# Expert attention: the low-part product of the two widest query tiles made in the two row halves of the array

## The reference

```
def _moe2_ref(x, w_gate, wq, wk, wv, wo):
    ...
    for e in range(E):                       # E = 4, for both batches
        q = x @ wq[e]
        k = x @ wk[e]
        v = x @ wv[e]
        scores = scale * (q @ k.transpose(0, 2, 1))
        causal = np.triu(np.ones((S, S), dtype=bool), 1)
        scores = np.where(causal, -1000000000.0, scores)
        scores = scores - scores.max(-1, keepdims=True)
        a = np.exp(scores)
        a /= a.sum(-1, keepdims=True) + 1e-09
        ye = a @ v @ wo[e]
        ...
```

## Time and profile before

| | before |
|---|---|
| median of three runs | 709.78 us (708.51 to 711.83) |
| the profiled execution: its time / its span | 710.88 us / 709.0 us |
| TensorE busy (matmuls) | 677.2 us (96%), 3808 instructions |
| VectorE busy | 356.4 us (50%), 828 |
| ScalarE busy | 393.9 us (56%), 800 |
| GpSimd busy | 273.9 us (39%), 244 |
| granted TensorE clock, mean | 0.998 of full speed (2.4 GHz), no slice lower than 9 tenths |

### The profile page before, as it was taken

The page is one execution under the profiler, slowest core; times in us unless marked ns, Lnnn a source line. Parts: engine busy times, 40 slices in busy tenths (PEclk is TensorE's granted clock), DMA queues, the critical chain, the costliest instruction groups (busy, mean ns, idle before and its releaser), DMA issues. The chain is left out here.

```text
span 709.0 us, 11959 instructions
## 1 busy us (share of the span) xinstructions
PE 677.2 (96%) x3808; PEld 538.7 (76%) x3808; DVE 356.4 (50%) x828; ACT 393.9 (56%) x800; POOL 273.9 (39%) x244
## 2 busy tenths in 40 slices
PE   6899999999999989999999999999999979999987
PEld 5677676677676737888888888888888968788866
DVE  5787778788788736111121111211112667786482
ACT  4777777777777746323343333433333656676574
POOL 6355454555444021444544444444443012232020
PEclk9999999999999999999999999999999999999999
DMA  4222111232120892000000000000000000000102
GB/s 150 61 92 86 60 63 61 64 105 65 60 63 16 239 306 60 0 0 0 0 1 0 0 0 0 0 0 0 0 0 1 30 1 1 0 1 31 60 2 89
DMA packets 26923, 31.34 MB, mean 44 GB/s; under 512 B 9664, under 2 KB 20880, under 8 KB 26896
## 3 DMA queue, kind: packets, MB, share of 16 engines
q1 hardware_dynamic: 26896, 31.01, 14.0%
HBM read 26.75 MB, written 3.15 MB: 42 GB/s over the span
## 5 line engine op out<-in xcount | busy, mean ns | idle before, releaser
L911 DVE SCALAR_TENSOR_TENSOR hid_l<-psT,hid_h 128x512 fp32r<-128x512 f32 x48 | 33.2, 692 | 212.1 <-ACT hid_h L887 212.1
L935 POOL TENSOR_TENSOR w_l<-w_raw,w_h 128x512 fp32r<-128x512 f32 x48 | 62.0, 1291 | 134.5 <-ACT w_h L878 134.5
L436 ACT ACTIVATE probs<-psS,scale_bias 128x768 f32<-128x768 f32 x96 | 95.2, 992 | 33.3 <-DVE scale_bias L522 32.8
L512 DVE TENSOR_REDUCE negmax<-psS 128x1 f32<-128x768 f32 x96 | 91.6, 954 | 30.2 <-PE psS L343 27.6
L356 PE MATMUL psT<-ident,probs 128*128 128x128 f32 x576 | 83.5, 276 | 3.7 <-ACT pt L445 1.8
L878 ACT ACTIVATE w_h<-w_raw 128x512 fp32r (+1 forms) x48 | 30.3, 631 | 95.2 <-PE psS L844 95.2
L356 PEld LDWEIGHTS psT<-ident,probs 128*128 128x128 f32 x576 | 66.6, 140 | 20.4 <-issue 9.6
L342 PE MATMUL psS<-k_hh,q_lh 128*128 128x384 f32 x192 | 73.9, 385 | 5.0 <-ACT probs L436 2.8
L833 PE MATMUL psT<-x_h,w_h 128*128 x192 | 74.8, 390 | 0.7 <-DVEq L903 0.7
L833 PE MATMUL psT<-x_l,w_h 128*128 x192 | 74.8, 389 | 0.0
L833 PE MATMUL psT<-x_h,w_l 128*128 x192 | 74.8, 389 | 0.0
(11 more groups left out here) (192 smaller groups left out, 1388.2 us busy)
## 6 DMA issues: line engine op xcount, KB each, us to landing
raw<-qk SPq DMA_DIRECT2D x15, 768.0 KB, 4.5
w_raw<-w SPq DMA_DIRECT2D x16, 256.0 KB, 6.7
w_raw<-w SPq DMA_DIRECT2D x4, 1024.0 KB, 8.6
raw_v<-v_n SPq DMA_DIRECT2D x16, 192.0 KB, 2.3
out<-y_out SPq DMA_DIRECT2D x11, 256.0 KB, 2.0
raw<-qk SPq DMA_DIRECT2D x2, 384.0 KB, 3.9
q_hb<-bits SPq DMA_DIRECT2D x30, 18.0 KB
k_lb<-bits SPq DMA_DIRECT2D x30, 18.0 KB
```

Of the source, the lines that this page charges most:

```text
L436: nc.scalar.activation(probs[j % 3][:].rearrange("p (c n) -> p c n", c=2), psS[:, score_slot(p, j), :, 0:HALF], ACT.Exp, bias=scale_bias[: ...
L512: nc.vector.tensor_reduce(negmax[:, p, j:j + 1], psS[:, score_slot(p, j), :, 0:HALF], AXIS.XY, ALU.max, negate=True).then_inc(rowmax_ready, 1)
L935: nc.gpsimd.tensor_tensor(w2_l[s][:].rearrange("p a b -> p (a b)"), w2_raw[:, f, :], w2_h[s][:].rearrange("p a b -> p (a b)").bitcast(F32) ...
```

## The change

For heads 1 to 7 and tiles 4 and 5, the products with `k_ll` no longer run over all 128 rows, twice in succession. The one for the first 512 keys uses rows 0 to 63 alone (high q times low k), and right behind it the one for the other 256 keys uses rows 64 to 127 alone, written to the second bank. The built instructions are placed in the array's upper and lower row half (64 x 128 each). Since rows 64 to 127 of `q_hl` hold the low part of q, a copy of the rounded q is made for these rows: `q_low`, 384 tokens (tiles 3 to 5), one more ScalarE instruction at the head of `round_qk` for c = 1. The product of the two low parts, which the 128-row form added for these tiles, is left out. Head 0, whose q comes from the stage before, and tiles 0 to 3 stay as they were.

```diff
@@ expert_attention
         summed = sb("esummed", [P, QT, D])
+        q_low = [sb(f"eq_low{p}", [P, HALF], F32R) for p in range(2)]
...
@@ scores
                         ps = psS[:, slot, c, 0:k.stop - k.start]
-                        nc.tensor.matmul(ps, q_hl[p][:, q], k_ll[p][:, k], start=True, stop=False)
+                        if j < 4 or h == 0:
+                            nc.tensor.matmul(ps, q_hl[p][:, q], k_ll[p][:, k], start=True, stop=False)
+                        elif c == 0:
+                            nc.tensor.matmul(ps, q_hl[p][0:D, q], k_ll[p][0:D, k], start=True, stop=False)
+                            other = slice(512, max(768, width))
+                            nc.tensor.matmul(psS[:, slot, 1, 0:other.stop - 512], q_low[p][D:P, q.start - HALF:q.stop - HALF],
+                                             k_ll[p][D:P, other], start=True, stop=False)
                         here = j // 4 == c
                         last = nc.tensor.matmul(ps, q_hl[p][:, q], k_hh[p][:, k], start=False, stop=not here)
...
@@ round_qk
                     act.wait_ge(qk_ready, 2 * (h - 1) + c + 1)
+                    if c == 1:
+                        nc.scalar.activation(q_low[h % 2][D:P, :], psS[0:D, c, 1, 0:HALF], ACT.Copy, scale=SCALE)
                     round_projection(nc, c, psS, q_hl[h % 2], k_hh[h % 2], False).then_inc(qk_rounded, 1)
```

## The result

| | before | after |
|---|---|---|
| median (lowest to highest) | 711.25 us (708.51 to 712.39), 13 runs | 714.06 us (712.91 to 718.25), 13 runs |
| the profiled execution: time / span | 710.88 / 709.0 us | 714.06 / 712.2 us |
| TensorE busy | 677.2 us, 3808 instructions | 680.3 us, 3808 |
| ScalarE busy | 393.9 us, 800 | 398.1 us, 807 |

The ratio is 1.0044, with the interval 1.0026 to 1.0062: slower by 3.1 us, or by 2.8 between the medians. The forecast was 711.3 us, in a range from 708.3 to 713.8; the measured median lies 0.3 us above that range.

The account below looks back on a forecast made before the run. VectorE was taken to bound heads 1 to 4 and 6, tile 4 and 5 score products heads 5 and 7. Terms 0.85 + 0.2 + 0.5 = +1.5 us gave 711.3 us from the median, range 708.3 to 713.8.

Parts of the forecast that it names:

- the starting point: Whole kernel: the +1.5 us sum was carried from the profiled execution's 710.88 us to the median of 709.78.
- the copy: ScalarE, heads 1 to 7: one added 0.49 us copy, mostly hidden by idle time; +0.5 us, 0.4 of it in head 0.
- the tiles: TensorE, tiles 4 and 5: +0.85 us at four exposed tiles in heads 5 and 7, +0.2 us in five VectorE-bound heads.
- without overlap: Rival: the row halves run one after the other in tiles 4 and 5, the gain absent; 712.8 us, chance 0.13.
- a full stop: Rival: TensorE drains at each change of shape in tiles 4 and 5, 0.58 us per tile; 717.0 us, chance 0.10.
- The slack of 0.42 us: ScalarE's idle time before tile 1's copy in head 3, said to hide all but 0.07 us of the added copy.
- The shape's round trip: TensorE, tiles 4 and 5: full array to halves and back, taken as 0.33 us from the hashed attention's column halves.
- the columns saved: TensorE, tiles 4 and 5: the 256-column product vanishes behind the 512-column one, saving 0.115 us per tile.
- The 0.2 for the five other heads: VectorE-bound heads: tile 4 fits 0.23 us of idle time, tile 5 overruns by 0.05 each; +0.2 us.
- the halves' start within 0.05 us: Sign in the profile after: the 256-column half product starts less than 0.05 us after the 512-column one.
- tile 5's 0.8 to 0.95 us in head 3: Sign: time from first low product to transposes; 0.75 if the shape change is free, over 1.2 at a stop.
- wrong if head 3 grows by over 0.3 us: Test refuting the forecast, alongside tiles 4 and 5 of head 5 getting shorter.

Follow-up runs that it names:

- e4: Kernel before plus only the added ScalarE copy, written to the rows it was read from (0 to 63); 711.1 against 710.62 us, ratio 1.0007.
- e8: Kernel before plus only the added ScalarE copy, placed between the roundings of q and k; 712.67 against 711.63 us, ratio 1.001.
- e6: Kernel before with only the 512-column low product of tiles 4 and 5 on rows 0 to 63; 713.75 against 710.75 us, ratio 1.0045.
- e7: Kernel before with both low products of tiles 4 and 5 on rows 0 to 63, a full product between; 719.55 against 710.75 us, ratio 1.0136.
- e3: Changed kernel without the copy, both half products in rows 0 to 63, one after the other; 714.82 against 710.62 us, ratio 1.006.
- e2: Changed kernel without the ScalarE copy, the second bank's half product taking q's low part instead; 712.94 against 710.62 us, ratio 1.0035.
- e1: Kernel before plus only the added ScalarE copy, ahead of both roundings, its result unused; 713.91 against 710.62 us, ratio 1.0037.
- e5: Changed kernel with q_low copied by GpSimd from q_hl instead of by ScalarE; 714.32 against 710.75 us, ratio 1.0067.
- e12: Changed kernel with the ScalarE copy placed between the roundings of q and k; 714.66 against 711.63 us, ratio 1.0042.
- a2: Changed kernel run once more, unaltered, for another profile; no half clock at 612 us but two other stretches; no median given.

## Why the prediction was wrong

**The direction and the mechanism hold**: slower, through both parts that were costed, none of them free. The distance from 711.3 to 714.06 us is 2.8: 1.5 for the starting point, 0.9 for the copy, 0.1 for the tiles, and 0.3 that no term explains. That the median lies between the rivals without overlap (712.8) and with a full stop (717.0) speaks for neither: the halves overlap, and a round trip costs less than the stop.

**The starting point, 1.5 us.** The sum was carried over to a median of three runs, 709.78; thirteen runs have 711.25. The profiled execution's 710.88, which the prediction put 1.1 us above the median, was nearer to it. With it the forecast would have been 712.4, as the prediction itself says. This part is the spread of the runs and says nothing on the mechanism.

**The step that failed: the added ScalarE copy, 0.5 us, measured 1.4.** Its length was right, 0.49 us, and so was that head 5 hides it (head 7 makes no copy). The error is the price of the place where it was put. I took its own duration, 0.49 us, as what it moves its successors by. But an instruction that keeps both overlaps with its neighbours moves them by only 0.37 (e4), and this one ends both, 0.12 to 0.13 us each, and moves them by 0.62. The slack of 0.42 us, compared with 0.49, left 0.07 to overrun, and that was covered; compared with 0.62 it leaves 0.20, and 0.14 to 0.16 of it arrive in each of heads 1, 3, 4 and 6; head 2 pays 0.23 instead of 0.07, and head 0 0.55 instead of 0.4. e8 shows that the rest of the reckoning was sound: with the copy where it costs 0.49, it measures 0.41 in head 0, 0.08 in head 2 and nothing in the others, the 0.4, 0.07 and 0 of the prediction.

**The tiles, 0.85 + 0.2 us, measured 1.09 + about 0.1 beside the copy** (1.65 without it). The shape's round trip was taken as 0.33 from the column halves and is 0.34 to 0.41 (e6, e7); the columns saved were taken as 0.115 and are 0.10 to 0.13 (e3 less e2). Net 0.21 per tile became 0.22 to 0.30. The other split of the array gave a price for this one within 0.08 us. The 0.2 for the five other heads looks right only by luck: without the copy, whose delay covers it, they lose about 0.6 us (e2). The Trainium skill (TensorEngine Tiling (Array Packing), Key Properties) says that a change of the tiling mode drains TensorE. The traces agree that each change costs, with 0.34 to 0.41 us for the way there and back, under the 0.58 of the full stop. Of the signs, the halves' start within 0.05 us and tile 5's 0.8 to 0.95 us in head 3 came true; heads 5 and 7 grew by 0.59 and 0.50, not 0.4, head 0 by 0.55, not 0.4, and heads 1 to 4 and 6 by 0.14 to 0.23 instead of staying within 0.1. What the prediction put as "wrong if head 3 grows by over 0.3 us" did not happen beside the clock: it grew by 0.19.

**What is left.** The trace gives 2.5 us, the ratio 3.1 (1.8 to 4.4). The ratios say more than the trace in nearly all experiments, and in e1 (1.5 to 3.7 against 1.35), e5 (3.4 to 6.1 against 2.1) and e7 (8.1 to 11.2 against 7.9) the trace lies below their intervals. Part of that may be the half clock: in e1's batch 11 of 12 executions with the copy had a mean clock of 0.995 or less, and 9 of the 29 of before, whose medians are 712.25 us for these nine and 710.98 us (at 0.997) and 710.56 us (at 0.998) for the rest. But in the same batch it is 7 of 12 in e2 and 5 of 12 in e4, and in e12's batch 8 of 12 against 19 of 29, so that the copy brings such stretches is not shown. Nor is it the whole: the four executions of the kernel after at 0.998 took 713.2 to 713.6 us. What starts them stays open, as does why e2's five executions at 0.998 (710.50) are no slower than before's at that clock (710.56), against 1.65 us in its profile.

**A version that beats both** was not found. One exposed tile gives up 0.34 to 0.41 us for 0.10 to 0.13; with the copy's cost gone as well (e2) the tiles alone are 1.65 us slower in the trace.

## What to carry to other kernels

A split of the array in row halves pays only where enough half products stand together to earn the round trip: 0.34 to 0.41 us here, against 0.11 for one 256-column product. An instruction that is squeezed into a slack costs what it moves its successor by, not its own length: read start-to-start distances of neighbours with the same rows, in and out, and with others, before comparing with an idle time nearly as long. A sum of small terms should be tied to the profiled execution rather than to a median of three, when the median's own error is as large as the sum.

## What the runs showed of the hardware

- **ScalarE's overlap depends on the rows of its neighbours.** A 64x384 copy out of PSUM follows another with the same rows in and out after 0.37 us (e4). Where the two write different rows it is 0.49 to 0.50 us (copy to q in e1, the two copies of k in the kernel before). Where the rows read differ and not those written it is 0.50 as well (copy to k in e8), but there the scale differs too, so the rows read are not shown as the cause. Behind an accumulator read it starts after 0.09 us, or after 0.22 where it reads rows 0 to 63 and writes 64 to 127.
- **The price of the array's shape adds up by the boundary**: one round trip 0.34 to 0.41 us (e6), two 0.73 to 0.80 (e7), in neither with any columns saved.
- **A GpSimd copy held up VectorE's small instructions.** The addition's 0.17 us became 0.64 (e5) and the gate choice's 0.17 became 0.44 (in the kernel before), each until GpSimd was done. The Trainium skill (SBUF — State Buffer, SBUF: two separate sides) says that VectorE and GpSimd share one pair of ports as an exclusive lock, and that a VectorE operation in a two-port mode is blocked for the whole of GpSimd's instruction where that starts first. The ends, 0.03 and 0.05 us apart, agree; in which mode the two ran no run shows. Not every instruction is held: the sum of the gates (L1029) kept its 0.18 us beside the same copy in e5.
- **Half clock in the expert heads.** The granted clock fell to 0.5 for 3 to 4 us at about 571, 580 or 612 in the profiles of the kernel after, a2, e1, e5, e8 and e12, at different places in two executions of the same kernel. A stretch costs 0.8 to 1.6 us, up to half of the difference measured here. All six kernels copy q to rows 64 to 127, and the six profiles without such a copy (before, e2, e3, e4, e6, e7) and the two with fillers show none; but in a2, e5, e8 and e12 one begins at 570 to 574, ahead of the first such copy at some 577 or later, which so can't be its cause. One profile per kernel doesn't settle it.
